# A four-byte tensor is allocated before the gate buffers instead of after them

## The reference

```python
w = softmax(weight_gen, over the 7 taps)              # per token and head, 8 heads of 24 columns
x = sum_k w[..., k] * x_padded[s + k]                 # window attention over the last 7 tokens
h = x @ w_in1;  g = h * np.cos(h);           x = g @ w_out1     # 192 -> 2048 -> 192
h = x @ w_in2;  g = np.maximum(0.01 * h, h); x = g @ w_out2     # 192 -> 2048 -> 192
```

## Time and profile before

| | |
|---|---|
| median of three runs | 1209.11 us |
| profiled execution | 1208.17 us |
| its span, first to last instruction | 1206.4 us |
| TensorE matmuls busy | 1167.8 us (97%), 10188 instructions |
| weight loads busy | 1036.5 us (86%) |
| VectorE busy | 910.9 us (76%) |
| ScalarE busy | 732.1 us (61%) |
| GpSimd busy | 117.4 us (10%) |
| mean granted TensorE clock | 0.992 |

### The profile page before, as it was taken

The page is one execution under the profiler, slowest core; times in us unless marked ns, Lnnn a source line. Parts: engine busy times, 40 slices in busy tenths (PEclk is TensorE's granted clock), DMA queues, the critical chain, the costliest instruction groups (busy, mean ns, idle before and its releaser), DMA issues.

```text
span 1206.4 us, 23265 instructions
## 1 busy us (share of the span) xinstructions
PE 1167.8 (97%) x10188; PEld 1036.5 (86%) x10188; DVE 910.9 (76%) x845; ACT 732.1 (61%) x789; POOL 117.4 (10%) x81
## 2 busy tenths in 40 slices
PE   8899889999999999999999999999999999999998
PEld 6678778898998889998898889989898888889876
DVE  7989887687876869677686977769687676977532
ACT  3767556574756657566575756657575665747544
POOL 4865310000000000000000000000000000000000
PEclk9899899999999999999999999999999999999999
DMA  9021100101001010100101010010100101000000
GB/s 243 27 82 54 33 1 2 47 2 47 1 14 34 1 47 1 47 2 1 47 1 47 1 44 4 1 47 1 47 1 14 34 1 47 1 14 1 1 14 27
DMA packets 10661, 32.68 MB, mean 27 GB/s; under 512 B 836, under 2 KB 5314, under 8 KB 10304
## 3 DMA queue, kind: packets, MB, share of 16 engines
q1 hardware_dynamic: 10560, 31.19, 8.1%
HBM read 24.89 MB, written 6.29 MB: 26 GB/s over the span
## 4 chain that ended last, share of the span: by engine, by line
PE 84%; DVE 8%; POOL 3%; ACT 3%; issue 1%; ACTq 0%; POOLq 0%
PE slot L915 37%; PE acc_a L915 26%; PE acc_b L915 17%; DVE g_lo L678 3%; DVE prods L277 2%; PE slot L1086 2%; ACT g_hi L523 2%; POOL prods L277 1%; DVE gate L742 1%; DVE prods L271 1%; POOL prods L271 1%; POOL out_hi_lo L464 0%; DVE gate L756 0%; PE slot L835 0%; POOL out_hi_lo L462 0%
## 5 line engine op out<-in xcount | busy, mean ns | idle before, releaser
L915 PE MATMUL acc_a<-g_hi,out_hi_lo 64*128 64x512 f32 x2000 | 700.6, 390 | 16.1 <-DVE prods L277 16.1
L678 DVE TENSOR_TENSOR g_lo<-gate,g_hi 128x1024 fp32r<-128x1024 f32 x256 | 322.1, 1258 | 188.5 <-ACT g_hi L523 188.5
L915 PEld LDWEIGHTS acc_a<-g_hi,out_hi_lo 64*128 64x128 f32 x2000 | 368.6, 185 | 45.0 <-issue 18.4
L915 PE MATMUL acc_b<-g_hi,out_hi_lo 64*128 64x512 f32 x1000 | 391.7, 392 | 7.7 <-DVE g_lo L678 5.7
L915 PE MATMUL acc_b<-g_lo,out_hi_lo 64*128 64x512 f32 x1000 | 388.1, 388 | 0.0
L915 PE MATMUL acc_a<-g_lo,out_hi_lo 64*128 64x512 f32 x1000 | 387.9, 388 | 0.0
L523 ACT ACTIVATE g_hi<-gate 128x1024 fp32r<-128x1024 f32 x256 | 271.4, 1060 | 132.6 <-PE acc_b L915 110.1
L915 PE MATMUL slot<-x_a_hi,in_a_lo 64*128 64x512 f32 x1000 | 300.1, 394 | 4.0 <-DVE gate L756 3.8
L915 PE MATMUL slot<-x_a_lo,in_a_hi 64*128 64x512 f32 x1000 | 297.1, 389 | 0.0
L915 PE MATMUL slot<-x_b,in_b_hi 64*128 64x512 f32 x1000 | 297.1, 388 | 0.0
L915 PE MATMUL slot<-x_a_hi,in_a_hi 64*128 64x512 f32 x1000 | 296.4, 388 | 0.0
(11 more groups left out here) (98 smaller groups left out, 1128.2 us busy)
## 6 DMA issues: line engine op xcount, KB each, us to landing
x_win<-in_x SPq DMA_DIRECT2D x14, 960.0 KB
out<-result SPq DMA_DIRECT2D x16, 384.0 KB, 2.3
raw_out<-in_moe_w_out SPq DMA_DIRECT2D x1, 1536.0 KB, 20.8
raw<-in_moe_w_out SPq DMA_DIRECT2D x4, 384.0 KB, 3.3
raw_in_a<-in_moe_w_in SPq DMA_DIRECT2D x1, 1024.0 KB, 13.1
raw_in_b<-in_moe_w_in SPq DMA_DIRECT2D x2, 512.0 KB, 15.6
raw<-in_moe_w_in SPq DMA_DIRECT2D x2, 512.0 KB, 6.3
raw<-in_moe_w_in SPq DMA_DIRECT2D x4, 256.0 KB, 4.0
```

Source lines behind the costliest of these rows:

```text
L678: nc.vector.tensor_tensor(g_lo[:, q % 2, :], gate[:, q % 2, :], g_hi[:, q % 2, :].bitcast(FP32), ALU.subtract)\
L915: return nc.tensor.matmul(to, w[rows, :], x[rows, :], start=start, stop=stop)
```

## The change

The allocation of `spare` moves from behind `g_lo` to between `whole` and `gate`.

```diff
         ident = sb("ident", [P, P])
         whole = sb("whole", [P, 2, PAIR * N], INT32)
+        spare = sb("spare", [1, 1])
         gate = sb("gate", [P, 2, PAIR * N])
         g_hi = sb("g_hi", [P, 2, PAIR * N], FP32R)
         g_lo = sb("g_lo", [P, 2, PAIR * N], FP32R)
-        spare = sb("spare", [1, 1])
```

## The result

The changed kernel takes 1229.16 us in the median of four runs (1229.11 to 1229.75), beside 1209.19 us of the kernel before in the same session. The ratio is 1.0162, with a 95% interval from 1.0141 to 1.0181: 1.6% slower, by 20 us, from four bytes. The forecast was 1209.1 us.

The account below looks back on a forecast made before the run. The prediction took TensorE's own pace to bound the kernel. All its terms were taken as 0, so the profiled 1206.4 + 1.8 = 1208.2 us, which stood 0.94 us under the median, gave 1209.1 us, range 1205 to 1224 us.

Parts of the forecast that it names:

- What bounds the kernel: Whole kernel: TensorE's own pace sets the end, 226.8 ns a pair, 250 stretches of 4.31 us, 1077 of 1206.4 us.
- term 1: TensorE reading the moved `g_hi` and `g_lo`, 3060 pairs: taken as 0, at most 20.4 us with 64-byte blocks.
- Term 2: VectorE's 512 instructions on the moved tensors: taken as 0, between 0 and 0.7 us on the path.
- term 3: ScalarE's instructions on the moved tensors (L523, L616, L584): taken as 0, at most 0.3 us on the chain.
- Term 4: Once-only work, GpSimd's memset of `g_hi` and the write of `spare`: 0, at most 15 ns more for the memset.
- The rival of longer fetch blocks: TensorE's moving reads in aligned 64-byte blocks delay each `g` stream: up to 21.4 us slower, 1230.5 us; chance 0.18.
- The rival of clashing streams: Weight load and `g_hi` stream contend at equal starts; the shift parts them: 13.8 us faster, 1195 us; chance 0.10.
- The rule of 16-byte lines: SBUF read in 16-byte lines: 32 bytes is two whole lines, so lines per operand stay the same and the sum is 0.
- The chances: Whole-kernel outcome: no change 0.68 (1206.7 to 1211.5 us), slower 0.22, faster 0.10.

Follow-up runs that it names:

- the bench of full products: Kernel before with groups of 30 products appended behind its end at further chosen starts; weights 0, moving 256 locked into 226.7 ns after ten products.
- the first bench: Kernel before with groups of 40 products or pairs of halves appended at chosen starts; full products took 226.7 ns at 0/0, 233.5 with moving at 32.

## Why the prediction was wrong

- *What bounds the kernel* was right: TensorE's pace, with little to hide a slower one. The loss of 21.1 us sits in the stretches, and the idle time of the other engines was of no use.
- *The step that failed is term 1*, "I take 0. The row nearest to it is VectorE's". The true term is about 115 ns for a stretch without waits and +21.1 us in all. The term was also laid on the wrong pairs: it counted the 12 of 19 that stream `g_hi` or `g_lo`, and the trace shows the x pairs slower too, 231.8 ns instead of 226.7. A row of VectorE says nothing on how TensorE's own two reads get on with each other. I had the relevant sight in front of me: all pairs took exactly the same 227 ns, and all of TensorE's operands had the same remainder by 512. Such a uniform row shows one point of a curve and no more.
- *Term 2 and term 3* were right: the medians of VectorE's and ScalarE's instructions moved by 1 ns at most, reads and writes alike, and the two places of `gate` that were compared cost the same. *Term 4* was right: the memset takes 952 ns instead of 950, the write of `spare` 203 instead of 202.
- *The rival of longer fetch blocks* gave 1230.5 us, 1.3 us from the truth, by luck: its mechanism is wrong. Its own mark, `g` pairs at 230 ns or more while x pairs stay at 226, failed in the trace after (x pairs 231.8 ns), and moving everything by 32 refuted it. Its 6.7 ns for a pair is also what a mismatched product costs in the bench (233.3 - 226.7 = 6.6 ns), again by chance as far as the runs show. A price that fits is not a mechanism shown.
- *The rival of clashing streams* named the right pair of accesses, the weight load and the stream that runs with it, and the wrong sign: equal starts are the good case (226.7 ns), and the shift is what costs.
- *The rule of 16-byte lines* from the Trainium skill, "SBUF — State Buffer", section Specifications (TRN2), gave 0 for this shift; the measurement is 1.6%, and it decides. The same page, in its section "A bandwidth-pool intuition that's wrong (but worth ruling out)", gives TensorE an independent second read port for weight loads. The runs differ: with only weights moved the kernel loses 2.0%, so the two reads are not independent in time.
- *The chances* were the smaller fault: 0.22 on slower, where the trace had no row for the one access on the bottleneck. The range ended at 1224 us because I trimmed the dear end of a rival whose bound I had worked out as 1230.5.

What stays open: what in the chip has the period of 256 bytes; why equal starts at 16 are slow; why the loss changes with the length as it does and turns the sign at 256 columns; why a pair with one mismatched half can run at full pace; and the exact share of a product's own and the next product's weights. That a disturbance can last up to ten products was seen in the bench of full products, and that changes between the kinds cost something was seen for pairs of halves in the last group of the first bench. That this is why the x pairs of the changed kernel are slow is an inference from the two: the kernel changes kind within 19 pairs and may never lock.

## What to carry to other kernels

Where TensorE sets the time with float32r products of 512 columns, keep the SBUF starts of all its moving and stationary operands at the same remainder by 256 bytes, and at multiples of 32; a small tensor in the middle of the list breaks this, at its end or padded to 256 bytes it doesn't. At 256 columns the bench showed the opposite sign, so for other lengths measure first. After any edit to allocations compare the start addresses of TensorE's operands and the step between matmul starts, not durations or busy shares. And where the bottleneck engine meets an access that no row shows, no row of another engine should shrink its bound.

## What the runs showed of the hardware

- The step of back-to-back float32r products of 512 columns is 226.7 ns when the starts of weights and moving operand have the same remainder by 256 bytes (tried at 0, 32, 64 and 96). Of the differences tried, 32, 96, 128 and 192 bytes cost 232 to 234 ns, and moving 64 bytes ahead costs 229. A start four bytes off (L1135 of the first bench) is the worst, 9.46 / 40 = 236.5 ns.
- After a disturbance the matched case needs 3 to 10 products to lock (steps between 224 and 236 ns until then).
- In pairs of halves, one mismatched half beside a matched one settles at 226.7 ns (L1141 of the first bench).
- In the kernel the loss ranges from 0.9% (only `g_hi`) to 2.0% (all weights), and none of the starts tried was faster than that of the kernel before.
